# Routed transformer block on one core: the rows of three chunks leave the first FFN untransposed, and their routing logits move from TensorE to VectorE

## The reference, cut to what matters

```python
attn_out = _attn_ref(q, k, v)                  # 4 batches, 8 heads, 576 tokens, 64 wide, block-causal
x = attn_out as rows                           # 2304 tokens x 512

h = x @ w_in                                   # first FFN: 512 -> 2048 -> 512
x = (h - np.tanh(h)) @ w_out

do_compute = x @ w_skip > 0                    # second FFN: routed, 8 experts of 512 -> 1024 -> 512
logits = xc @ w_gate                           # xc: the tokens with do_compute
e_idx = np.argmax(logits, axis=1)              # one expert for a token
gate_w = softmax(logits)[e_idx]
out = x;  out[do_compute] = xc + gate_w * (relu(xc @ w1[e]) @ w2[e])
```

## Time and profile before

| | us |
|---|---|
| median of 3 runs | 818.54 |
| lowest and highest | 815.25, 820.29 |
| the profiled execution's own time | 817.64 |
| its span, first to last instruction | 816.0 |
| TensorE busy | 796.6 |
| VectorE, ScalarE, GpSimd busy | 434.6, 303.7, 251.2 |

### The profile page before, as it was taken

How to read it: one execution, slowest core, us unless ns; L and a number is a source line. 1 busy time by engine, 2 the same in 40 slices (tenths; PEclk the granted TensorE clock), 3 DMA queues, 4 the chain that set the end, 5 groups by cost and what they waited for, 6 DMA issues and landing times.

```text
span 816.0 us, 14983 instructions
## 1 busy us (share of the span) xinstructions
PE 796.6 (98%) x4744; PEld 623.4 (76%) x4745; DVE 434.6 (53%) x1026; ACT 303.7 (37%) x750; POOL 251.2 (31%) x307
## 2 busy tenths in 40 slices
PE   5999999999999999999999999999999999999996
PEld 3556555556888888888888888888998888888885
DVE  4878788786343324334333343324467656656653
ACT  3777677674101211103111121112216245645642
POOL 4766767667850000100010000100031333233333
PEclk9999999999999999999999999999999999999999
DMA  9243444421310001000010001000154176665664
GB/s 182 69 112 85 99 103 115 113 57 40 104 53 0 1 1 52 1 0 1 15 37 0 0 0 39 14 1 0 41 124 160 58 256 196 221 199 173 210 208 141
DMA packets 82722, 66.90 MB, mean 82 GB/s; under 512 B 62682, under 2 KB 62682, under 8 KB 82672
## 3 DMA queue, kind: packets, MB, share of 16 engines
q1 hardware_dynamic: 77728, 60.56, 25.7%
q0 software_dynamic: 3760, 5.38, 1.9%
q10 hardware_dynamic: 1184, 0.30, 0.2%
HBM read 60.59 MB, written 8.83 MB: 85 GB/s over the span
## 4 chain that ended last, share of the span: by engine, by line
PE 78%; DMA 11%; issue 5%; POOL 2%; DVE 2%; POOLq 1%; ACT 0%; ACTq 0%; DVEq 0%
PE psum L1289 45%; PE psum L1259 6%; PE psum L1237 6%; PE psum L1208 6%; DMA xg<-out_dram,rec_next 5%; DMA out_dram<-y_rows,rec_now 4%; PE psum L1456 3%; PE psum L1193 3%; PE psum L1481 2%; PE psum L1374 2%; PE psum L1461 1%; PE psum L1486 1%; PE psum L1382 1%; DMA xg_third<-out_dram,rec_early 1%; DMA lists<-rec,slot_i 1%
## 5 line engine op out<-in xcount | busy, mean ns | idle before, releaser
L1033 DVE TENSOR_TENSOR g<-psum,g 128x512 f32<-128x512 f32 (+1 forms) x80 | 51.1, 638 | 246.2 <-ACT g L755 246.1
L755 ACT ACTIVATE g<-psum 128x512 f32<-128x512 f32 (+1 forms) x80 | 44.5, 556 | 322.4 <-PE psum L1289 320.3
L541 POOL DMA_INDIRECT lists<-rec,slot_i x18 | 18.5, 1025 | 355.0 <-DVE slot_i L967 351.0
L1289 PE MATMUL psum<-g_hi,wo_hi 128*128 128x512 f32 (+1 forms) x320 | 118.1, 369 | 0.4 <-DVE g_lo L1037 0.3
L1289 PE MATMUL psum<-g_hi,wo_lo 128*128 128x512 f32 (+1 forms) x320 | 117.8, 368 | 0.0
L1289 PE MATMUL psum<-g_lo,wo_hi 128*128 128x512 f32 (+1 forms) x320 | 117.7, 368 | 0.0
L516 POOL TENSOR_SCALAR probs<-probs,row_inv 128x384 f32<-128x384 f32 (+2 forms) x96 | 99.1, 1042 | 59.0 <-DVE row_inv L856 59.0
L1289 PE MATMUL psum<-x_hi,wi_hi 128*128 128x512 f32 x256 | 102.6, 401 | 0.0
L1289 PE MATMUL psum<-x_lo,wi_hi 128*128 128x512 f32 (+1 forms) x256 | 101.1, 395 | 0.0
L1289 PE MATMUL psum<-x_hi,wi_lo 128*128 128x512 f32 x256 | 100.8, 394 | 0.0
L658 ACT ACTIVATE probs<-psum,neg_max 128x576 f32<-128x576 f32 (+2 forms) x144 | 74.7, 527 | 21.0 <-DVE neg_max L849 17.9
(11 more groups left out here) (208 smaller groups left out, 1282.9 us busy)
## 6 DMA issues: line engine op xcount, KB each, us to landing
w_half<-in_moe_w_dram SPq DMA_DIRECT2D x64, 512.0 KB
q_rows<-in_q_dram SPq DMA_DIRECT2D x32, 144.0 KB, 3.0
out_dram<-x_rows SPq DMA_DIRECT2D x18, 256.0 KB
k_rows<-in_k_dram SPq DMA_DIRECT2D x30, 144.0 KB, 3.1
v_rows<-in_v_dram SPq DMA_DIRECT2D x32, 128.0 KB, 2.3
w_raw<-in_moe_w_in_dram SPq DMA_DIRECT2D x16, 256.0 KB, 3.4
w_raw<-in_moe_w_out_dram SPq DMA_DIRECT2D x16, 256.0 KB, 2.5
v_rows<-in_v_dram SPq DMA_DIRECT2D x32, 16.0 KB, 2.2
```

What stands on the lines that cost most here:

```text
L1033: dve.tensor_tensor(g_f, h_at(f, first, last), g_f, ALU.subtract).then_inc(g_done, 1)
L1289: mm = pe.matmul(dst, w, m, start=(first and n == 0), stop=(last and n == 2), skip_group_check=True)
```

## The change

Chunks 0 to 2 swap the operands of `output`: g is stationary, the weights move. The same number of products of the same width gives x2 by rows, a tile of 128 tokens in each bank. ACT copies these banks straight to `x2_rows`, from where SP stores them. `logits` and `turn_rows` of these chunks are gone. Their nine scalars for each token come from `dots`, run by DVE in the next chunk: 36 operations in a chunk (nine columns by four tiles), three in each of the steps 0 to 11, each a product of 128x512 elements with a column of weights that stands alike on all partitions, summed along the row into `r_logit`. The products themselves are thrown away, by turns into a free bank and a free part of `x_t`. `choose` and `rank` move to steps 12 and 13 and `place_tokens` to 14. Chunk 3 still comes out transposed; in chunk 4 its logits are computed a tile at a time between the other products, and its rows are turned as before. SP has new transfers: the columns of `w_gate` and `w_skip` are written as nine rows to a DRAM tensor `w_rows`, and each row is later loaded to all partitions (nine loads of 256 KB). POOL clears two buffers after the lists of chunk 2 instead of ahead of all lists.

```diff
+    DOTS, CHOICE = 3, 12
+    ALL_DOTS = NR * (NE + 1)
...
+    wide_x2 = placer(X2_AT)("wide_x2", [P, KC, DM], F32)
+    wide_raw = placer(RAW_AT)("wide_raw", [P, 2, DM], F32)
+    wide_w = [wide_x2[:, n, :] for n in range(KC)] + [wide_raw[:, n, :] for n in range(2)] + \
+             [x_t[:, TOK * n:TOK * n + DM] for n in range(NE + 1 - KC - 2)]
...
+        unused = [turn_ps, x_t[:, TOK * (KC - 1):TOK * (KC - 1) + DM]]
...
+            with nc.allow_non_contiguous_dma("4096 words of w_gate"):
+                sp.dma_start(w_rows[0:NE], moe2_w_gate.rearrange("d e -> e d")).then_inc(w_rows_in, 16)
+            sp.dma_start(w_rows[NE:NE + 1], moe2_w_skip.rearrange("(o d) -> o d", o=1)).then_inc(w_rows_in, 16)
             load_values(sp, 1)
             load_pair(2)
...
+            def load_wide(ns):
+                for n in ns:
+                    sp.dma_start(wide_w[n], w_rows[n:n + 1, :].to_broadcast([P, DM])).then_inc(wide_in, 16)
+
+            sp.wait_ge(w_rows_in, 32)
+            load_wide(range(0, KC))
             for n in range(PAIRS, 2 * PAIRS):
                 load_raw(n)
+            sp.wait_ge(raw_used, 2 * PAIRS)
+            load_wide(range(KC, KC + 2))
+
+            sp.wait_ge(h_done, FT)
+            load_wide(range(KC + 2, NE + 1))
...
-            pool.wait_ge(raw_used, 2 * PAIRS)
+            with pool.Fori(0, BY_ROWS) as c:
+                list_tokens(c)
+            pool.wait_ge(dotted, ALL_DOTS * BY_ROWS)
             for i in range(EARLY - 1):
                 pool.memset(xg_early[i][:], 0.0).then_inc(early_zero, 1)
-            with pool.Fori(0, NCH - 1) as c:
-                list_tokens(c)
+            list_tokens(BY_ROWS)
...
-                for d in range(KC):
-                    high((rest_t if last else x2_t)[:, d, :], acc_ps[:, d, 0:n]).then_inc(x2_out, 1)
+                if last:
+                    act.wait_ge(x2_turned, NR)
+                elif not first:
+
+                    act.wait_ge(dotted, ALL_DOTS * c)
+                if last or to_rest:
+                    for d in range(KC):
+                        high((rest_t if last else x2_t)[:, d, :], acc_ps[:, d, 0:n]).then_inc(x2_out, 1)
+                else:
+                    act.wait_ge(rows_free, c + 1)
+                    for t in range(NR):
+                        high(x2_rows[:, t, :], acc_ps[:, t, :]).then_inc(x2_out, 1)
...
+            def dots(c, f):
+
+                if f == 0:
+                    dve.wait_ge(wide_in, 16 * (NE + 1))
+                    dve.wait_ge(x2_out, KC * c + KC)
+                for n in range(DOTS * f, DOTS * f + DOTS):
+                    e, t = n // NR, n % NR
+                    if n >= 2:
+
+                        dve.wait_ge(dotted, ALL_DOTS * c + n - 1)
+                    dve.scalar_tensor_tensor(unused[n % 2], x2_rows[:, t, :], 1.0, wide_w[e], ALU.mult, ALU.mult,
+                                             accum_out=r_logit[:, t, e:e + 1]).then_inc(dotted, 1)
...
-                    if f == 3 and not first:
+                    if not first and not last:
+                        if f < CHOICE:
+                            dots(c - 1, f)
+                        if f == CHOICE:
+                            choose(c - 1, by_rows=True)
+                        if f == CHOICE + 2:
+                            place_tokens(c - 1)
+                    if f == 3 and last:
                         choose(c - 1)
...
+                gh, gl = g_at(g_hi, f, last), g_at(g_lo, f, last)
+                if last or to_rest:
+                    for d in range(KC):
+                        wh, wl = wo_hi[:, f, P * d:P * d + P], wo_lo[:, f, P * d:P * d + P]
+                        mm = three(acc_ps[:, d, 0:w], ((wh, gh), (wh, gl), (wl, gh)), f == 0, f == FT - 1)
+                else:
+                    for t in range(NR):
+                        th, tl = gh[:, RT * t:RT * t + RT], gl[:, RT * t:RT * t + RT]
+                        wh, wl = wo_hi[:, f, :], wo_lo[:, f, :]
+                        mm = three(acc_ps[:, t, :], ((th, wh), (tl, wh), (th, wl)), f == 0, f == FT - 1)
...
+                    if last and f in (2, 3):
+                        logits(c - 1, tiles=(2 * f - 4,))
                     if f >= 2:
-                        output(c, f - 2, first, last)
-                    if not first:
-                        if f == 2:
-                            logits(c - 1)
+                        output(c, f - 2, first, last, to_rest)
+                    if last:
+                        if f in (2, 3):
+                            logits(c - 1, tiles=(2 * f - 3,))
                         if 3 <= f < 3 + NR:
                             turn_rows(c - 1, f - 3)
                         if f == 5:
                             rank(c - 1)
-                        if f == 5 and last:
                             count(r_sofar[:, NR, :], counted_early)
+                    elif not first and f == CHOICE + 1:
+                        rank(c - 1)
```

66 lines of the change are left out of this document (39 added, 27 removed).

## The result

The changed kernel takes 832.73 us, the median of 4 runs (829.9 to 835.17), the kernel before 819.41 in the same batch (4 runs, 815.25 to 821.27). The ratio is 1.0171, 95% interval 1.0133 to 1.0209: slower by 1.3 to 2.1%, where 799.2 and a range up to 806 had been forecast. The profiled execution took 831.37 us, its span is 829.7.

A forecast was written before the change was run, and what follows sets the result against it. TensorE's instruction list was taken to bound the chunks; 10.8 + 5.3 + 3.2 = 19.3 us off a profiled 817.64 gave 798.3, plus 0.9 for the median: 799.2 us. Range 795 to 801, with rivals 795 to 806.

The forecast's parts named there:

- SP's new transfers: At the start, ahead of turn 2's keys: 4096 words take 3.2 to 4.9 us, under 6.7 available; cost 0.
- The words of w_gate hold up turn 2: Rival at turn 2's keys: TensorE waits, 803 to 808 us, or 842 through one engine; 10%, 1% of it single engine.
- The FFN's sum: First FFN: logits gone 10.8, transposes gone 5.3 and clock 3.2, together 19.3 us off.
- 3.59 for the logits: Chunks 1 to 3: each row of logits removed from TensorE saves 3.59 us, three times, 10.8 us.
- 4 x 0.44 for the transposes: Chunks 1 to 3: each transpose group removed from TensorE saves 0.44 us, 12 times, 5.3 us.
- Clock: Behind the logits in chunks 1 and 2: low-clock products cost 1.6 us each time; 3.2 us regained, ends 0 and 4.8.
- Swapped operands: `output` in three chunks, 576 products with g as weights: nothing added, ends -1.2 and +1.2 us.
- VectorE, 0.8 us a sum: Three sums in a step at 0.8 us each: 4.2 us of VectorE inside TensorE's 5.48; range 0.692 to 1.54 a sum.
- rival from 1.23 on: Steps 0 to 12, chunks 1 to 3: VectorE becomes the bound; at 1.54 us a sum, 33 us lost, 832; 6%.
- Choice and ranking: Steps 12 and 13: counts are ready for `rank` with 0.4 us to spare; 0, at the end 0.9 us.
- ScalarE, GpSimd, chunk 4: ScalarE loses 12 copies, GpSimd's lists come eight steps later, chunk 4 reorders products; 0, its 1.5 us gathered-tile wait stays.

The follow-up runs named there:

- words_late: Changed kernel with both transfers into `w_rows` issued behind the last load of FFN weights; 798.03 us, ratio 0.9725 to the kernel before.
- sixteen: Changed kernel with its one transfer taking the words in the order in which they lie in w_gate, successive words 2 KB apart; 797.88 us, ratio 0.9761.
- words_sbuf: Kernel before plus 4096 single words, 32 bytes apart in `moe_w_in`, read to SBUF at the change's place; 817.44 us, ratio 0.9981.
- tiles: Kernel before with every chunk's logits computed a tile at a time, runs of 8 nine-column products instead of 32, no work removed; 814.39 us, ratio 0.9953.
- before_words: Kernel before with only the two transfers into `w_rows` added at the change's place, read by nobody; 855.97 us, ratio 1.0426.
- words_act: Changed kernel with the transfer of the 4096 words issued on ScalarE's queue instead of SP's; 846.72 us, ratio 1.037.

## Why the prediction was wrong, step by step

**SP's new transfers: this step failed.** I put 0, with "4096 over 16 engines are 256 each: 3.2 to 4.9 us, under 6.7". It cost 34.1 us. The keys of turn 2 are turned at 54.94 us instead of 23.71, 31.2 us later. The other 2.9 us come right behind: TensorE ran the first products at the low level, 1.2 GHz, after it had stood idle. The same products begin at 29.09 us before and at 63.22 after, 34.1 us later, like the first product of the first FFN:

```profile
29.09 0.66 PE L1208 MATMUL psum<-ident,probs 128*128 128x128 f32 x4
```

```profile
63.22 0.66 PE L1280 MATMUL psum<-ident,probs 128*128 128x128 f32 x4
...
54.00:60.00 6.00, 5.06 (x24) 2.97 (x28) 1.45 (x5) 1.84 (x6) 2.50 (x3) 0.50 0.61 119
```

The mechanism and its place were named (SP's queue, the keys of turn 2), and so was the rival: "The words of w_gate hold up turn 2", priced at 803 to 808 us, or 842 through a single engine. It got 10%, and its wait, 3.5 to 8.7 us, was put four to nine times too small. Two terms were wrong. The engines were 8 and not 16, so "an outer dimension of 4096 that can be spread" was one side of the transfer only; by itself that would have given 512 x 12 to 19 ns, 6.1 to 9.7 us, and at most 3 us of wait. The larger error is the price of a packet. In `words_late`, from 232 to 274 us, 4280 packets take up 43.1% of 16 engines for 42 us, 68 ns each; I had computed with 12 to 19.

```profile
q1 hardware_dynamic: 4280, 0.28, 43.1%
```

The prices came from rows that were unlike in what decided: the earlier trace rows reads 256 bytes, and the earlier trace rows writes 8 bytes, but 128 of them in eleven microseconds and scattered. The sentence that "no row shows 4-byte writes side by side in DRAM" was there, and the range should have followed from it: an operation with no row near it that stands ahead of all loads of the next turns has no upper end. `sixteen` shows how little it would have taken for the step to be right: 3.4 us blocked, no wait for the keys of turn 2 beyond 0.3 us.

The Trainium skill's rules that I cited speak against the transfer, and they were right to; but `sixteen` and `words_sbuf` have the same packets of 4 bytes, so they can't tell the cheap order from the dear one.

**The FFN's sum: 19.3 forecast, 20.0 measured.** Per chunk: 3.59 for the logits, 4 x 0.44 for the transposes and 1.6 for the clock are 6.95; measured are 94.87 - 87.85 = 7.02. Chunk 3, without a dip in the profile before, and what changed in chunk 4 leave 20.0 - 2 x 7.02 = 6.0, where 5.35 had been written.

- *Clock, 3.2 (0 to 4.8):* 1.00 in all windows. `tiles` takes the long runs away and nothing else, in chunk 4 too, and gains 4.8 by the medians (2.2 to 5.5). That the sum came out so near rests on luck in part: the profile before had two dips, and others with the same first FFN have one or three.
- *Swapped operands, 0:* 73.73 / 324 = 0.228 us, unchanged.
- *VectorE, 0.8 us a sum, rival from 1.23 on:* 0.61 from start to start, below my lower end of 0.692, because the next instruction starts before the last one's end. The rival's case (1.54) didn't come near.
- *Choice and ranking, "0.4 us to spare":* the last count ends at 387.52 and `rank` starts at 387.97, 0.45 us.

```profile
386.75 0.77 DVE L1009 TENSOR_TENSOR r_sofar<-r_sofar,r_one 128x8 f32<-128x8 f32 x4
...
387.97 0.30 PE L1471 MATMUL psum<-r_one,before 128*128 128x32 f32 x2
```

- *ScalarE, GpSimd, chunk 4, 0:* no new wait; the one for the gathered tile is 1.3 us after 1.5. For chunk 4 the term wasn't quite nothing: its run of 32 was cut up as well, and other profiles of the old code show a dip there.

The gain was passed on to the stages behind in full. The three versions without the stall, 797.18, 797.88 and 798.03 us, lie within 2.1 us of the 799.2 forecast, and beat both kernels.

## What to carry to other kernels

A transposing copy of single words in DRAM isn't priced by its bytes: look at its order and at the outermost dimension of both sides. Write it so that successive words go far apart and the outermost dimension isn't the short one (here one `rearrange` did both, 832.73 to 797.88 us), or issue it where nobody waits: behind the loads or a column at a time between the turns (798.03 and 797.18 us). Where an added transfer has no row like it in the trace, measure it alone in the old kernel before the rest is judged; one run of `before_words` would have shown all 36 us. And read a slower total by stages first: here a gain of 20 us, close to the 19.3 computed, lay behind a loss of 34.

## What the runs showed of the hardware

- One transfer of 4096 words, column after column of a 512x8 matrix, written side by side in DRAM, used 8 engines and took 42 us with no other load issued (`words_late`); in the matrix's own order it used 16 and landed in 9.7 us, with other loads around it (`sixteen`).
- On 8 engines, the wait behind such a transfer fell with the distance of successive words: 34.4, 19.8, 10.9 and 2.4 us at 4, 16, 32 and 64 bytes. On 16 engines side by side it was 6.7 to 8.2 us.
- The instruction behind it on the issuing queue is blocked for 28 to 31 us, and loads on another queue are held up as well (20.06 us in `words_act`).
- A product with a sum along the row is two instructions of VectorE, 0.69 us and 0.08 or 0.14 us, but costs 0.61 us from start to start for 128x512.
- Behind 3.5 us of back-to-back nine-column products, with no idle time, the granted clock fell to 0.50 for a few products, in 27 of 39 places; runs of 8 (0.8 us) between wide products never did that.
